# A two-phase MLP-mixer kernel: first phase in blocks of 512 tokens, scores and values on quarters of the array

## What is computed

```python
# q, k, v: (8, 8 heads, 576, 64), in 9 chunks of 64 tokens
scores = scale * q_c @ k_c.T;  scores -= max(scores)
attn = exp(scores);  attn /= sum(attn) + 1e-9
x = attn @ v_c                                   # -> (8, 576, 512)
h = relu(x.T @ w_tok1) @ w_tok2                  # tokens 576 -> 256 -> 576
u = x + h.T
x2 = u + relu(u @ w_ch1) @ w_ch2                 # channels 512 -> 1536 -> 512
h = relu(x2 @ w_in);  a, v = halves of h         # 512 each
v_n = (v - mean) / sqrt(var + 1e-6)
out = (a * (w_spatial @ v_n + b_spatial)) @ w_out
```

## Time and profile before

| | us |
|---|---|
| median of three runs | 1360.96 |
| lowest and highest of them | 1359.4, 1361.09 |
| profiled execution | 1359.22 |
| its span | 1357.4 |

### The profile page before, as it was taken

One profiled execution on the slowest core, in us unless ns is written; L12 is line 12 of the kernel. 1 busy time (PEld: TensorE's weight loads), 2 busy tenths in 40 slices (PEclk: granted clock), 3 DMA queues, 4 the chain that ended last, 5 costly groups with the idle time before them and its releaser, 6 DMA issues.

```text
span 1357.4 us, 26091 instructions
## 1 busy us (share of the span) xinstructions
PE 1343.2 (99%) x9485; PEld 1291.7 (95%) x9485; DVE 528.3 (39%) x1167; ACT 418.6 (31%) x843; POOL 64.2 (5%) x45
## 2 busy tenths in 40 slices
PE   9999999999999999999999999999999999999998
PEld 9999999999999999999999999999998998998997
DVE  3343234234224324423432342234563463463461
ACT  6532133123213312321321331123433433433332
POOL 3800000000000000000000000122000000000000
PEclk9999999999999999999999999999999999999999
DMA  9523021212302211220230210312021021021002
GB/s 251 127 53 67 21 42 42 40 38 40 66 22 44 54 26 43 55 45 25 53 67 21 42 34 1 130 47 90 1 87 55 0 76 63 0 70 70 1 1 70
DMA packets 183429, 70.57 MB, mean 52 GB/s; under 512 B 159184, under 2 KB 171088, under 8 KB 183312
## 3 DMA queue, kind: packets, MB, share of 16 engines
q1 hardware_dynamic: 183312, 68.98, 20.2%
HBM read 50.05 MB, written 18.87 MB: 51 GB/s over the span
## 4 chain that ended last, share of the span: by engine, by line
PE 99%; issue 1%; ACT 0%; POOL 0%; POOLq 0%
PE bank L1053 31%; PE bank L1206 23%; PE bank L1188 23%; PE bank L1131 5%; PE bank L1115 5%; PE bank L1071 4%; PE bank L1144 3%; PE bank L1106 1%; PE bank L1079 1%; PE bank L1122 1%; PE bank L1225 1%; PE bank L1149 0%; PE bank L1148 0%; PE bank L1082 0%; PE bank L1165 0%
## 5 line engine op out<-in xcount | busy, mean ns | idle before, releaser
L832 DVE SCALAR_TENSOR_TENSOR hidl<-bank,hidh 128x256 fp32r<-128x256 f32 (+1 forms) x192 | 88.0, 458 | 438.6 <-ACT hidh L649 438.6
L1206 PE MATMUL bank<-hidh,w2h 128*128 128x256 f32 (+1 forms) x768 | 237.1, 309 | 0.0
L1188 PE MATMUL bank<-uh,w1h 128*128 128x256 f32 (+1 forms) x768 | 228.3, 297 | 7.8 <-issue 7.8
L1188 PE MATMUL bank<-uh,w1l 128*128 128x256 f32 (+1 forms) x768 | 227.3, 296 | 0.0
L1188 PE MATMUL bank<-ul,w1h 128*128 128x256 f32 (+1 forms) x768 | 227.3, 296 | 0.0
L1206 PE MATMUL bank<-hidh,w2l 128*128 128x256 f32 (+1 forms) x768 | 227.1, 296 | 0.0
L1206 PE MATMUL bank<-hidl,w2h 128*128 128x256 f32 (+1 forms) x768 | 226.7, 295 | 0.0
L649 ACT ACTIVATE hidh<-bank 128x256 fp32r<-128x256 f32 (+1 forms) x192 | 78.9, 411 | 456.6 <-PE bank L1188 456.6
L1188 PEld LDWEIGHTS bank<-uh,w1h 128*128 128x128 f32 x768 | 145.8, 190 | 9.9 <-issue 9.3
L1206 PEld LDWEIGHTS bank<-hidh,w2h 128*128 128x128 f32 x768 | 145.4, 189 | 1.6
L1206 PEld LDWEIGHTS bank<-hidl,w2h 128*128 128x128 f32 x768 | 145.6, 190 | 0.5
(11 more groups left out here) (158 smaller groups left out, 2356.7 us busy)
## 6 DMA issues: line engine op xcount, KB each, us to landing
x2l_raw<-x_scratch SPq DMA_DIRECT2D x32, 256.0 KB, 4.3
out<-out_tile SPq DMA_DIRECT2D x32, 256.0 KB, 2.0
qn<-in_q SPq DMA_DIRECT2D x30, 256.0 KB, 3.2
vn<-in_v SPq DMA_DIRECT2D x30, 256.0 KB, 3.9
kn<-in_k SPq DMA_DIRECT2D x448, 16.0 KB, 1.7
x_scratch<-x_half SPq DMA_DIRECT2D x8, 640.0 KB, 4.2
x_scratch<-x_half SPq DMA_DIRECT2D x8, 512.0 KB, 3.3
w1l_raw<-in_moe_w_ch SPq DMA_DIRECT2D x6, 512.0 KB, 9.1
```

The lines of the kernel that those rows point to most:

```text
L832: return nc.vector.scalar_tensor_tensor(lo, src, 0.0, hi.bitcast(F32), op0=ALU.max, op1=ALU.subtract)
L1188: last = nc.tensor.matmul(hid_bank[g % 2][:, 0:width(h)], w, x, start=(c == 0 and e == 0), stop=(c == KC - 1 and e == 2))
L1206: last = nc.tensor.matmul(acc_bank[c][:, 0:n], w, x, start=(f == 0 and e == 0), stop=(f == KF - 1 and e == len(ops) - 1))
```

## The change

The first phase is rewritten; the second computes the same with the same lines.

- The 8 x 576 tokens are cut into 9 blocks of 512 that run over the bounds of the elements. An element's token-down product has two parts, UA for the block that it shares with the one before (512 - 64b columns of element b) and UB for the next (64 + 64b columns). UB of an element and the side jobs of the next one stand behind the groups of one block (`REST`, `PLAN`).
- A side job stands behind an up or a down group; the order of groups is up 0, up 1, down 0, up 2, down 1, and so on.
- SC and PV are 16 products of 64 x 64 in place of 8 (SC) or 8 (PV), each on a quarter of the array: row half e is the head of a pair, column half a is the chunk. The two row halves write to two PSUM banks. The transposed tiles of q, k and p hold no zeros, are copied once by ScalarE, and in the main part have one buffer in place of two.
- v is loaded in four transfers a tile, q in one, k in blocks as before. GpSimd adds ul (`add_low`), VectorE the rest of the residual. x2 shares its memory with uh and leaves in one transfer for each element that the block touches, two as a rule; ScalarE waits for the store before it writes uh again (UB).
- In the prologue VectorE multiplies by 1/sum in place of GpSimd, the memsets of q_t and p_t are gone, and the token-up products of each tile (MP) stand between the other jobs. The order of weight transfers is mixed with the second element's tiles.
- hidh and hidl have two buffers in place of three. All loops are written out.

```diff
+    BW = 512
+    NB = B * S // BW
+    def share(kind, b):
+        cut = BW - REM * b
+        return (0, cut, b, REM * b) if kind == "UA" else (cut, S, b + 1, 0)
+    GROUPS = [("up", 0), ("up", 1)]
+    for f in range(KF):
+        GROUPS += [("down", f)] + ([("up", f + 2)] if f + 2 < KF else [])
+    PLAN = {0: "TQ.0", 1: "SC.0", 2: "TQ.1", 3: "PT.0", 6: "SC.1", 7: "PV.0", 8: "PT.1 TQ.2", 9: "SC.2", 10: "PV.1",
+            11: "PT.2 TQ.3", 12: "SC.3", 13: "PV.2", 14: "PT.3 TQ.4", 15: "SC.4", 16: "PV.3", 17: "PT.4", 18: "PV.4",
+            19: "M.0", 20: "M.1", 21: "UA.0 UA.1", 22: "UA.2 UA.3"}
+    REST = {4: "UB.0 UB.1", 5: "UB.2 UB.3"}
...
+    PRO_PE = jobs(0, "TQ.0 TK.0 TQ.1 TK.1 SC.0 TQ.2 TK.2 SC.1 PT.0 TQ.3 TK.3 PV.0 SC.2 PT.1 TQ.4 TK.4 PV.1 SC.3 PT.2 "
+                     "PV.2 SC.4 PT.3 MP.0 PV.3 PT.4 MP.1 PV.4 MP.2 MP.3 M.0 M.1 UA.0 UA.1 UA.2 UA.3")
...
                 elif kind == "SC":
-                        for a in range(2 if t < KS else 1):
-                            c0 = (2 * g + a) * CHUNK
-                            last = nc.tensor.matmul(bank[:, c0:c0 + CHUNK], q_t[:, t % 2, g, a, :],
-                                                    k_t[:, t % 2, g, a * CHUNK:(a + 1) * CHUNK], start=True, stop=True)
+                        for e in range(2):
+                            for a in range(n // CHUNK):
+                                r, s = slice(e * D, (e + 1) * D), slice(a * CHUNK, (a + 1) * CHUNK)
+                                last = nc.tensor.matmul(two[s, e, g * CHUNK:(g + 1) * CHUNK], qt[r, g, s], kt[r, g, s],
+                                                        start=True, stop=True)
...
                 elif kind == "PV":
-                    for h in range(H):
-                        last = nc.tensor.matmul(bank[0:n, h * D:(h + 1) * D], p_buf(i, t)[0:n, h, 0:n],
-                                                nat_tile(i, "v", t)[:, h, :], start=True, stop=True)
+                    for g in range(PAIRS):
+                        for e in range(2):
+                            for a in range(n // CHUNK):
+                                r, s = slice(e * CHUNK, (e + 1) * CHUNK), slice(a * CHUNK, (a + 1) * CHUNK)
+                                last = nc.tensor.matmul(two[s, e, 256 + g * D:256 + (g + 1) * D], pt[r, g, s],
+                                                        vt[r, g, a, :], start=True, stop=True)
...
+            def token_down(kind, b, c, bank):
+                s0, s1, _, _ = share(kind, b)
...
+                        if a1 - a0 == P:
+                            nc.tensor.matmul(turned.bitcast(F32R), x[:, s, cs], rows_, is_transpose=True,
+                                             start=False, stop=False)
+                        else:
+                            nc.tensor.matmul(turned, x[:, s, cs], rows_, start=False, stop=False)
...
+            def add_low(j):
+                for c in range(KC):
+                    pool.wait_ge(acc_free, KC * j + c + 1)
+                    nc.gpsimd.tensor_tensor(x2[j % 2][:, c, :], x2[j % 2][:, c, :], ul[j % 2][:, c, :].bitcast(F32),
+                                            ALU.add).then_inc(x2_ready, 1)
...
+            def store_x2(j):
+                sp.wait_ge(x2_ready, KC * (j + 1))
+                for kind, b in (("UB", j - 1), ("UA", j)):
+                    if 0 <= b < B:
+                        s0, s1, _, at_ = share(kind, b)
+                        sp.dma_start(x2_dram[b, :, :, s0:s1],
+                                     x2[j % 2][:, :, at_:at_ + s1 - s0]).then_inc(x2_stored, DMA)
...
+                    if kind == "UB" and j >= 2:
+                        act.wait_ge(x2_stored, stored(j - 2))
...
-            with pe.Fori(0, B - 1) as i:
-                body(i, SIDE, False)
-            body(B - 1, LAST_SIDE, True)
+            for j in range(NB):
+                for g, (kind, f) in enumerate(GROUPS):
+                    if kind == "up":
+                        up(j, f)
+                    else:
+                        down(j, f)
+                    for job in behind(j, g):
+                        side_job(job)
```

More of the change, by code:

```diff
@@ L16, with jobs @@
 BLK = 32
[L19 to L28, removed]
+def jobs(b, text):
+    return [(kind, b, int(t)) for kind, t in (x.split(".") for x in text.split())]
 def build(nc, q, k, v, w_tok1, w_tok2, w_ch1, w_ch2, w_in, w_spatial, b_spatial, w_out, out, x2_dram):
@@ L119, in parts @@
-    def parts(i, job):
-        seq = order(i)
-        return sum(j[0] in TWO_PART for j in seq[:seq.index(job) + 1])
-    side_tally = Tally(len(PRO), len(BODY))
-    part_tally = Tally(sum(j[0] in TWO_PART for j in PRO), sum(j[0] in TWO_PART for j in BODY))
-    bank_tally = [Tally(len(PRO[b::PRO_BANKS]), len(BODY[b::2])) for b in range(2)]
-    tile_tally = Tally(NT, NT)
+    CW_EARLY = 2
+    TWO_PART = ("PV", "M", "UA", "UB", "WT", "WR")
+    SEQ = list(PRO)
+    for j in range(NB):
+        for g in range(NG):
+            SEQ += behind(j, g)
@@ new lines, in build, with tile_no @@
+    BANKS["M", 0, 0], BANKS["M", 0, 1] = (2,), (3,)
+    for job in SEQ[len(PRO):]:
+        one = {"TQ": 1, "PT": 0}.get(job[0], job[2] % 2)
+        BANKS[job] = (0, 1) if job[0] in ("SC", "PV") else (one,)
+    number = {job: n + 1 for n, job in enumerate(SEQ)}
+    parts = {}
+    for job in SEQ:
+        if job[0] in TWO_PART:
+            parts[job] = len(parts) + 1
+    in_bank = {n: [job for job in SEQ if n in BANKS[job]] for n in range(8)}
+    def tile_no(b, t):
+        return b * NT + t
@@ L518, in store_out @@
                                      out_tile[bb * REM:(bb + 1) * REM, n % 2, :]).then_inc(s, DMA)
-            def pair(j, last):
-                if not last:
+            for j in range(NP):
+                if j < NP - 1:
                     sp.wait_ge(full, j * NJ + job_no(("U", NU - 1)))
@@ L1008, in gate_low @@
                 r.then_inc(g_lo, 1)
-            def pair(j, last):
-                gates = [m for kind, m in PHASE2 if kind == "SP"]
+            dve.wait_ge(bias_loaded, DMA)
+            for j in range(NP):
                 for n in range(NJ):
@@ L1085, in side, with token_up @@
[L1085 to L1097 removed]
+            def token_up(t, bank, s):
+                cols = slice(t * P, (t + 1) * P)
+                for e, (w, x) in enumerate(three(t1h[:, s, cols], t1l[:, s, cols], xh[:, s, :], xl[:, s, :])):
+                    nc.tensor.matmul(bank, w, x, start=(s == 0 and e == 0), stop=False)
@@ L1183, in up @@
                 for c in range(KC):
                     if f == 0:
-                        pe.wait_ge(part_lo, part_tally.at(i, parts(i, (f"U{h}", c))))
-                    for e, (w, x) in enumerate(three(w1h[:, c, cs], w1l[:, c, cs], uh[:, c, ts], ul[:, c, ts])):
-                        last = nc.tensor.matmul(hid_bank[g % 2][:, 0:width(h)], w, x, start=(c == 0 and e == 0),
+                        pe.wait_ge(part_lo, parts["UA", j, c] if j < B else parts["UB", j - 1, c])
+                    for e, (w, x) in enumerate(three(w1h[:, c, cs], w1l[:, c, cs], uh[j % 2][:, c, :], ul[j % 2][:, c, :])):
+                        last = nc.tensor.matmul(hid[:, n % 2, :], w, x, start=(c == 0 and e == 0),
```

906 lines of the change are left out of this document (437 added, 469 removed), and 6 rows, old and new, of the table SIDE.

## The result

The changed kernel takes 1298.4 us, the median of 4 runs (1298.1 to 1301.6), and the kernel before 1360.7 beside it: a ratio of 0.9549, 95% interval 0.9533 to 0.9566. The forecast was 1298 us. That the number fits is partly luck: the scores and values gained some 25 us more than forecast, and five other terms, the prologue first among them, together cost some 25 us more. The profile shows where.

What follows compares the result with a forecast made beforehand. TensorE, busy 1343.2 of 1357.4 us, was taken to bound the kernel. The terms sum to -61.7 us, taking the profiled 1359.2 to 1297.5, stated as 1298 us, with a range of 1262 to 1346.

Steps and rivals of the forecast that it cites:

- MLP in blocks of 512: MLP matmuls: 2592 of 512 columns replace 2304 each of 256 and 320; 614.5 to 587.6 us, -26.9 us.
- loops: Batch loop written out: six gaps at its branch back go, -8.8 us; the second phase's loop gives nothing.
- quarters, 7 elements: Scores and values: two quarters work at a time, full tile 1.27 us instead of 1.79; -33.5 us, ends -63 and +25.
- token mixing: UA and UB: narrow column parts and extra transposes cost more; +8 us, between +3 and +34.
- waits at the transposes: Transposes of the probabilities at tiles 1 and 3 wait 0.25 us twice in 7 elements; +3 us, 0 to 7.
- last tile's transposes: The last tile's transpose of the probabilities takes 64 rows and pays the mode change; +1 us.
- prologue without its UA: Prologue: values end near 33.5 instead of 34.4, UA starts near 37.6 instead of 41.3; -4.5 us, between 0 and -8.
- the first rival: Scores and values: four quarters work at a time, -63 in place of -33.5, 1268 us; chance 0.12.
- the second (rows must differ): Scores and values: quarters overlap only where their rows differ, 1.73 us a full tile, -8 in all, 1323 us; chance 0.2.
- the third: Scores and values: quarters don't overlap, +25 in place of -33.5, 1356 us; chance 0.15.
- fourth: Scores and values: each change of quarter drains like a mode change, +112 in place of -33.5, 1443 us; chance 0.06.
- the fifth: Unseen stalls (late store, late code, narrow matmuls at fp32's price) on top of the forecast, 1305 to 1345 us; chance 0.1.

Runs made afterwards that it cites:

- unrolled: Kernel before the change with only its loops over batch elements and pairs written out; 1351.3 us, ratio 0.9934.
- norm_first: Changed kernel with VectorE's softmax normalisation before, not behind, the hidden group's residue in each MLP group; 1293.3 us, ratio 0.9513.
- turn_early: Changed kernel with VectorE's first turn of the second element's k moved ahead of block 0; 1296.6 us, ratio 0.9542.
- q_cols: Changed kernel with products reordered: all of one row half first, neighbours alternating in column half only; 1316.3 us, ratio 0.9676.
- all4: Changed kernel with norm_first, turn_early and, in the prologue, v transfers one tile later and values' low part before the next normalisation; 1292.5 us, ratio 0.951.
- adj_norm: norm_first with values of four of five tiles per element straight behind the next tile's scores, beside the MLP; 1282.0 us, ratio 0.9434.

## Why the prediction was right or wrong

The forecast, term by term, and what the runs and traces show for it:

```
term                       forecast  measured   from
MLP in blocks of 512         -26.9     -21      0.229 us a matmul on average: 2592 x 0.229 = 593.6
loops                         -8.8      -9.1    unrolled
quarters, 7 elements         -33.5     -58      8 x 0.83 + 2 x 0.81 = 8.3 an element, before 16.5
token mixing                  +8       +10.6    its lines, start to start: 78.0 before, 88.6 after
waits at the transposes       +3        +5.8    14 x 0.42, norm_first
last tile's transposes        +1        +1      7 x (0.59 - 0.45), start to start
stop and low clock, block 0    -        +3.8    2.2 + 1.6, trace; both gone in turn_early
prologue without its UA       -4.5      +6.4    56.2 - 45.7 = 10.5, of which 4.1 is UA
sum                          -61.7     -60.5    spans: -60.9
```

- **What bounds the kernel** was right: what a change takes off TensorE's stream is gained, and the six blocks without a mishap show each term.
- **The MLP** was mis-sized by 6 us. I took the 512-column spacing of the second phase, 0.2267, for all. Groups behind another MLP group or behind token-up products have it, as the twelve from 426.33 to 429.05 us. Behind any other side job up to ten of the next matmuls start up to 0.236 us apart, even past the longer first gap; behind a stay on the quarters the average is 0.229.
- **The quarters** failed at one step: "the two instructions of one product ... must follow each other at 0.058, while the next product ... can begin with the second of the one before." The first half holds. The second drew the wrong picture: not two neighbours but all four quarters run abreast, each with its own row of rounds. My own objection to the first rival, the two instructions of a product, costs nothing as long as three other quarters fill the time between. The bound of 0.80 for four at a time was measured as 0.82 to 0.83, and the half tile, 0.80, as 0.81. The forecast's end of -63 had the half tile, too, at four quarters, of which it uses two; -60 was the bound.
- **The rivals:** the first held in its step, though its 1268 us did not come: the prologue took 11 us more than it had, the MLP 6, its own -63 was 5 too much, block 0 lost 4, and token mixing and the transposes 3 each; the second (rows must differ) fell with q_cols; the third and fourth fell with the fours in the timeline. Part of the fifth came, as stalls of some 10 us, but none for a late store: 1024 KB landed in 4.8 us, and in the view of waits none of ScalarE's for a store stands ahead of UB.
- **Token mixing** was right within 3 us: after a 64-column matmul the next starts 0.11 us later, where I had 0.10.
- **The waits at the transposes** were right in place and mechanism; each of the 14 cost 0.42 us where the chain of durations gave 0.25.
- **The prologue** was the second failed step: "about the tile period of today. So values end near 33.5." Values ended near 42 us and UA began at 47.8, not near 37.6. I added up VectorE's passes and not the order they stand in, and I took the banks as free. The tile period became 7 us (scores at 18.97, 26.56 and 33.25 us), because three bank pairs in turn are freed only by the low part, because four transfers for a tile's v take 3.1 us of SyncE where I had looked only at the later elements' room, and because TensorE, half idle, lost its clock; what the clock alone cost no run separates. In all4 another limit, the weights' loads, held the first MLP group at the same 55 us.
- **Block 0** was not looked at by itself: its turn of k and GpSimd's work on the weights are in no other block.

What stays open: how much of the prologue's 6.4 us belongs to which limit. The order of VectorE and the transfers of v, each removed alone, gave less than the 2.4 us by which equal prologues differ. Also open is why the MLP's matmuls start further apart behind a side job.

## What to carry to other kernels

Small fp32 products on quarters of the array pay when neighbours in the queue stand on different quarters: with one quarter eight instructions long, 59 of the change's 62 us were gone. Do as much as possible between one entry into the quarters and the exit, since that pair costs some 0.36 us for one job as for two. A prologue is a pipeline of its own: its forecast needs the order of every queue and who frees which bank, and a sum of busy times is only its lower bound.

## What the hardware showed that I had not expected

- Four fp32 products on four quarters run at once, their instructions starting in fours every 0.058 us; two quarters that differ only in columns overlap as well as two that differ in rows (0.91 and 0.90 us a tile).
- With the same quarter eight instructions long, a tile of 32 takes 23 rounds and not 32. TensorE starts instructions on free quarters before others that stand ahead of them in its queue (adj_norm, 115.24 and 115.26 us).
- A VectorE step of 128 x 8 took 1.50 to 2.14 us instead of 0.17, and ended within 0.03 us of the GpSimd instruction beside it.
- At the same granted clock of 1.00, matmuls of 512 columns start 0.2267 us apart, but behind most side jobs up to ten of the next twelve start up to 0.236 us apart; no run here shows why.
